# First attention steps of a fused attention, MLP and routed-experts kernel: who normalises the first step, in which order its heads and values are loaded, and where the third step's values stand

## The reference

```python
B, H, S, D = 4, 8, 576, 64                       # q, k, v
scores = q @ k.T / sqrt(D) - slope[h] * |i - j|  # only 0 <= i - j < 128, else -1e9
attn   = exp(scores - rowmax); attn /= attn.sum(-1) + 1e-9
x      = (attn @ v) as (2304 tokens, 512)
h      = x @ w_in                                # 512 -> 2048
x      = (h * clip(h + 3, 0, 6) / 6) @ w_out     # 2048 -> 512
e      = argmax(cosine(x, expert_emb) / tau)     # 8 experts, gate = softmax value of e
out    = gate * (relu(x @ w1[e]) @ w2[e])        # 512 -> 1024 -> 512
```

## Time and profile before

| | |
|---|---|
| median of 3 runs | 838.8 us (838.38 to 839.31) |
| the profiled execution | 838.55 us, of which the span from first to last instruction is 836.8 us |
| PE busy | 823.3 us, 98% of the span |
| DVE, ACT, POOL busy | 477.9, 395.8, 241.5 us |
| first matmul of the MLP | 22.18 us after the span's start |

### The profile page before, as it was taken

How to read it: one execution, slowest core, us unless ns; L and a number is a source line. 1 busy time by engine, 2 the same in 40 slices (tenths; PEclk the granted TensorE clock), 3 DMA queues, 4 the chain that set the end, 5 groups by cost and what they waited for, 6 DMA issues and landing times.

```text
span 836.8 us, 18599 instructions
## 1 busy us (share of the span) xinstructions
PE 823.3 (98%) x6533; PEld 707.0 (84%) x6533; DVE 477.9 (57%) x1469; ACT 395.8 (47%) x1057; POOL 241.5 (29%) x261
## 2 busy tenths in 40 slices
PE   7999999999999999999999999999999999999996
PEld 6888888888888888888888888888888888888885
DVE  7765575665766656756565578776543445554000
ACT  5674555545455455554554337533434334343442
POOL 5992000000000000000000101386665656666432
PEclk9999999999999999999999999999999999999999
DMA  8764211102112111121100026575555444552100
GB/s 243 226 190 152 77 52 58 33 15 76 52 41 69 33 40 51 52 76 35 32 13 2 27 88 168 167 224 176 165 161 169 128 140 140 164 157 66 50 14 11
DMA packets 54427, 80.18 MB, mean 96 GB/s; under 512 B 11752, under 2 KB 28136, under 8 KB 54210
## 3 DMA queue, kind: packets, MB, share of 16 engines
q1 hardware_dynamic: 47986, 67.57, 26.6%
q0 software_dynamic: 4000, 11.29, 4.2%
q10 hardware_dynamic: 2352, 0.14, 0.3%
HBM read 69.51 MB, written 11.30 MB: 97 GB/s over the span
## 4 chain that ended last, share of the span: by engine, by line
PE 94%; DMA 2%; DVE 2%; issue 0%; ACT 0%; SPq 0%; POOL 0%; POOLq 0%; ACTq 0%; DVEq 0%
PE ps_h L852 24%; PE ps_y L869 22%; PE ps_h L1004 16%; PE ps_s L1033 15%; PE ps_out L797 4%; PE ps_s L755 3%; PE ps_y L1028 3%; PE ps_out L1033 1%; PE ps_out L956 1%; DMA y_scratch<-gate_tok 1%; PE ps_s L774 1%; DMA arena<-in_k 1%; PE ps_s L780 1%; PE ps_s L777 1%; DMA en_all<-y_scratch,gather_ids 0%
## 5 line engine op out<-in xcount | busy, mean ns | idle before, releaser
L852 PE MATMUL ps_h<-x_hi,win_hi 128*128 128x256 f32 x576 | 165.6, 295 | 0.1
L852 PE MATMUL ps_h<-x_lo,win_hi 128*128 128x256 f32 x576 | 158.5, 283 | 0.0
L852 PE MATMUL ps_h<-x_hi,win_lo 128*128 128x256 f32 x576 | 158.3, 283 | 0.0
L1160 ACT CAST gated_hi<-gated 128x256 fp32r<-128x256 f32 x144 | 58.5, 406 | 138.3 <-PE ps_y L869 98.4
L1428 DVE TENSOR_TENSOR gated_lo<-gated,gated_hi 128x256 fp32r<-128x256 f32 x144 | 64.6, 449 | 101.9 <-ACT gated_hi L1160 101.9
L852 PEld LDWEIGHTS ps_h<-x_hi,win_hi 128*128 128x128 f32 x576 | 107.8, 190 | 8.3 <-issue 2.7
L869 PE MATMUL ps_y<-wout_hi,gated_hi 128*128 128x512 f32 x288 | 114.1, 396 | 0.0
L869 PE MATMUL ps_y<-wout_hi,gated_lo 128*128 128x512 f32 x288 | 113.8, 395 | 0.0
L628 POOL MEMSET arena<- 128x64 bf16 x2 | 0.2, 151 | 390.8 <-DVE x_lo L1402 390.8
L869 PE MATMUL ps_y<-wout_lo,gated_hi 128*128 128x512 f32 x288 | 112.1, 389 | 0.0
L852 PEld LDWEIGHTS ps_h<-x_hi,win_lo 128*128 128x128 f32 x576 | 107.9, 191 | 2.3
(11 more groups left out here) (241 smaller groups left out, 1563.7 us busy)
## 6 DMA issues: line engine op xcount, KB each, us to landing
arena<-in_moe_w SPq DMA_DIRECT2D x64, 512.0 KB, 4.2
arena<-in_v SPq DMA_DIRECT2D x40, 128.0 KB, 3.2
y_scratch<-y_sb SPq DMA_DIRECT2D x9, 512.0 KB, 3.8
en_all<-in_moe_w_in SPq DMA_DIRECT2D x16, 256.0 KB, 3.9
arena<-in_v SPq DMA_DIRECT2D x16, 256.0 KB, 3.2
en_all<-in_moe_w_out SPq DMA_DIRECT2D x16, 256.0 KB, 3.9
arena<-in_q SPq DMA_DIRECT2D x31, 128.0 KB, 2.4
arena<-in_k SPq DMA_DIRECT2D x31, 128.0 KB, 2.9
```

The costliest lines, as they stand in the source:

```text
L852: last = pe.matmul(ps_h[m % 2][:, 0:TB], a[:, c, w], r[:, c, x], start=n == 0, stop=n == 3 * KC - 1)
L1160: act.copy(gh[m % 2][:], gate[:]).then_inc(act_gh, 1)
```

## The change

ACT instead of DVE multiplies the probabilities of step 0 by the reciprocals (`normalise_first`). DVE still computes the reciprocals (`invert(0)`), now ahead of the last four biases. SP issues v of group 0 ahead of q and k of step 3, then two weight pieces, v of group 1, q and k of step 4, and two more weight pieces; `start_at_one` comes after all of these. On PE, the scores of step 4 go from iteration 2 to behind the transposes of step 2 in iteration 3, the values of step 2 go ahead of the transposes of step 3, and the idle transposes are 6 and 8 around the values of step 1 and 3 ahead of the values of step 3.

```diff
@@ load order, SP @@
             load_qk(1)
             load_qk(2)
-            start_at_one(sp, counting)
+            load_v(0)
             load_qk(3)
             for n in range(4):
+                if n == 2:
+                    load_v(1)
+                    load_qk(4)
                 sp.dma_start(w_raw[n], w_piece(n)).then_inc(ld_w[n], 16)
-                if n == 0:
-                    load_v(0)
-                    load_qk(4)
-            load_v(1)
+            start_at_one(sp, counting)
@@ transposes, PE @@
-                pe.wait_ge(dve_n, s + 1)
+                if s == 0:
+                    pe.wait_ge(act_n, 1)
+                else:
+                    pe.wait_ge(dve_n, s)
@@ main loop, PE @@
-                if 2 < it < FIRST:
-                    keep_busy((3, 14)[it - 3])
-                    if it == FIRST - 1:
-                        transposes(it - 1)
-                    values(it - OUT)
-                    if it == 3:
-                        keep_busy(8)
-                if 0 <= it - 1 < STEPS and it != FIRST - 1:
+                if it == 3:
+                    keep_busy(6)
+                    values(1)
+                    keep_busy(8)
+                if it == FIRST - 1:
+                    values(2)
+                if 0 <= it - 1 < STEPS:
                     transposes(it - 1)
                 if it == 2:
                     values(0)
+                if it == 3:
                     scores(4)
+                if it == FIRST - 1:
+                    keep_busy(3)
@@ ACT @@
+            def normalise_first():
+                act.wait_ge(dve_r, 1)
+                for n in range(4):
+                    a = columns_of(0, n)
+                    last = act.activation(a, a, ACT.Copy, scale=rinv[0:rows(0), 0, n:n + 1])
+                last.then_inc(act_n, 1)
...
+                if it == 1:
+                    normalise_first()
                 if 0 <= it - 1 < STEPS and it != FIRST - 1 and not turn_first:
                     take_pT(it - 1)
@@ DVE @@
-            def normalise(s):
+            def invert(s):
...
                 dve.reciprocal(rinv[0:R, b, :], rden[0:R, b, :]).then_inc(dve_r, 1)
+
+            def normalise(s):
+                R, b = rows(place(s)[0]), s % 2
+                invert(s)
                 dve.wait_ge(dve_r, s + 1)
...
                 if it == 1:
+                    invert(0)
                     bias_before(4, H)
-                    normalise(0)
```

More of the change, by code:

```diff
@@ L358, in _program @@
         pe_s, dve_s, act_e = sem("pe_s"), sem("dve_s"), sem("act_exp")
-        dve_d, dve_r, dve_n = sem("dve_den"), sem("dve_inv"), sem("dve_norm")
+        dve_d, dve_r, dve_n, act_n = sem("dve_den"), sem("dve_inv"), sem("dve_norm"), sem("act_norm_first")
         pe_t0, pe_t, act_t0, act_t, pe_o = sem("pe_t0"), sem("pe_t"), sem("act_t0"), sem("act_t"), sem("pe_o")
@@ L1364, in scores @@
                         op0=ALU.add, op1=ALU.min, accum_out=nmax[0:R, s % 2, n:n + 1]).then_inc(dve_s, 1)
-            def normalise(s):
-                g, i, q4 = place(s)
-                R, b = rows(g), s % 2
+            def invert(s):
+                R, b = rows(place(s)[0]), s % 2
                 dve.wait_ge(act_e, 4 * s + 4)
```

## The result

The changed kernel takes 843.2 us (median of 6 runs, 841.97 to 844.6) where the kernel before takes 838.8 (6 runs, 838.19 to 839.31). The ratio is 1.0054, 95% interval 1.0041 to 1.0067: 4.4 us slower. The forecast was 838.0 with a range to 839.6, so it was wrong, in sign and in size.

What follows compares the result with a forecast made beforehand. The prediction took PE's gapless matmul queue to bound the kernel, so its start sets the end. With the MLP at T + 10.54, 0.7 to 1.3 earlier, it took 0.8 off 838.55, giving 837.75, plus 0.25: 838.0, range 836.9 to 839.6.

Steps and rivals of the forecast that it cites:

- Bottleneck and method: Whole kernel: PE's gapless middle bounds it, so an earlier MLP start should move the end by as much.
- the sum: MLP start is T + 10.54: 21.5 at T = 10.95, 0.7 earlier, or 20.85 at T = 10.3, 1.3 earlier.
- T + 10.54: From DVE's scores of step 2 to the MLP's first matmul: 10.54 us, where it was 11.39 before.
- T: Start of DVE's scores of step 2: forecast 10.95 or 10.3, by the pace of PE's scores of step 3; before 10.79.
- the heads of step 3 come too late: Rival at PE's scores of step 3: k lands after 9.5, at 10.0 the MLP starts 0.5 later, 839.3; chance 0.14.
- The chance of the clock: At PE's start: standing still from about 7.5 to 8.8 may keep full clock away; counted by leaning to 0.8 gained.
- The rival on the clock: PE behind 15.7: half clock slows scores of step 4 and values of step 2; 0.45 slower, 839.2; chance 0.17.
- The three waits of 0.85: PE's order ahead of the MLP: waits of 0.49, 0.20 and 0.16 would go, with values of step 2 in front.
- ACT's normalising: Step 0 on ACT: four multiplications taking 1.15, ending at 9.6, freeing DVE at about 9.9 instead of 10.79.
- The gain in T (0.54): At DVE's scores of step 2: ACT's normalising brings them to 10.25, before the new load order takes part back.
- Weights, v, `start_at_one`: Loads ahead of the MLP: weight pieces in time with 3.3 of room, v early enough, moving `start_at_one` costs nothing.

Runs made afterwards that it cites:

- e4: The changed kernel with 3 and 6 idle transposes put into PE's gaps ahead of the scores of steps 2 and 3; 840.15 us, ratio 1.0023.
- e8: The changed kernel with the heads of step 3 loaded ahead of v of group 0 and idle transposes in PE's gaps; 839.15 us, ratio 1.0004.
- e1: The changed kernel with the load order of the kernel before; 841.69 us, ratio 1.0031.
- e6: The kernel before with only ACT's normalising of step 0 and the reciprocals ahead of the biases; 839.43 us, ratio 1.0015.
- e15: The changed kernel without all 17 idle transposes; 843.49 us, ratio 1.0057.
- e7: The changed kernel with the old load order and without the 6 and 8 idle transposes; 840.94 us, ratio 1.0018.
- e3: The changed kernel with the heads (q and k) of step 3 loaded ahead of v of group 0; 840.71 us, ratio 1.0012.
- e2: The kernel before with the new load order alone; 842.11 us, ratio 1.0040.
- e16: The changed kernel as it is, run again on another chip; 842.77 us, ratio 1.0041.
- e5: The kernel before with PE's new order alone, on the slower chip; 844.92 us, ratio 1.0009.
- e14: The kernel before with PE's new order alone, on a faster chip; 839.86 us, ratio 1.0004.

## Why the prediction was wrong

Bottleneck and method held: 4.71 of the 5.0 us lie ahead of the MLP's first matmul, and each row behind it moved along. The MLP starts 5.4 later than the 21.5 of the sum (26.89). Term by term:

- **T + 10.54, the failed step (3.7 of the 5.4).** It is T + 14.21. The prediction put it: "the 6 wait for DVE's scores of step 3 (T + 2.23) and are done before x_lo of step 0, the 8 run while DVE still normalises step 2 [...]: nothing of them is on the path." All its durations on PE behind T were those of full clock. At half clock DVE waited 0.88 for the transposes of step 1, and the transposes of step 2 started 1.47 after their turn (20.10, not 12.68 + 5.07 + 0.88 = 18.63), behind the values of step 1 and the 8. From there to the transposes of step 3 it took 3.70, not 2.54, and the rest 0.16 more. 0.88 + 1.47 + 1.16 + 0.16 = 3.67.
- **T, 1.7 of the 5.4.** T is 12.68, forecast 10.95. The scores of step 3 started at 9.90 and not at 8.8: k was issued at 6.15 instead of 5.9 and landed 3.6 later instead of 2.9. It lay inside my bounds (2.3 to 4.1), and I chose too near the lower one. k landed after the 9.5 at which the rival "the heads of step 3 come too late" sets in, so that rival's condition came true; but its price, 0.5 us, was worked out at full clock behind T and is a ninth of the loss. The other 0.63 is the transposes of step 0: from their start to T it took 1.29 at half clock, where I had 0.64 for them.
- **The chance of the clock.** The prediction named what happened, in one sentence: PE "now stands still from about 7.5 [...] to 8.8, and the full clock that the row shows behind 8.9 may not come". But it priced it as 0.7 on one block of scores and followed it no further. The rival on the clock looked only behind 15.7 and took full clock until then. (Its upper bound is also too low by its own terms: 2 times 1.08 is 0.66 above the 1.5 that gave 839.2, so 839.9 and not 839.7. The 843.2 lies beyond either.) e4 shows the size of what was left out: 2.9 us.
- **The three waits of 0.85.** Their working was right at full clock. In e8 x_hi of step 1 does not wait, and the transposes of step 3 start at 18.89, 0.15 after their turn (x_hi of step 1 at 15.97, + 0.80 + 1.74 + 0.23): the values of step 2 do fit in front. e8 starts the MLP at T + 11.35 and not T + 10.54 because of a new wait of 0.56 on DVE (next point), these 0.15, and 0.17 behind them (18.89 to 21.99 is 3.10 for 2.93); 0.07 were won in between.
- **ACT's normalising.** 1.26, forecast 1.15, as good as right. The gain in T (0.54) did not come: T is 10.78, 10.89 and 10.64 in e1, e6 and e8, against 10.79. PE's transposes of step 0 start behind ACT at 9.75 or so, and T is their end. And what the prediction did not follow is ACT's next piece: the copy of these transposes comes later too, and DVE's scores of step 3 wait for what stands behind it, so x_hi of step 0 is at T + 2.73 to 2.79.
- **Weights, v, `start_at_one`**: as forecast, without a wait ahead of the MLP.

The Trainium skill (TensorE: Matmul & The Clock Gate, Part 4: PE-mode transpose) says that transposes do not count for the full clock as other matmuls do. The runs do not agree. In the changed kernel PE ran from 16.02 to 21.52 almost only transposes, and the full clock came within the scores that followed; with the idle ones taken away, in e15, it came some 2 us later. In e1 it rose at 17.1, in the middle of 8 idle transposes, and in e7, without them, at 20.9. The values of step 1 stand among these transposes, so no run here has them alone.

The scatter fits the mechanism, though no run proves it: on e1's chip 32 of the 35 runs of the kernel before lie within 1.9 us (838.0 to 839.9, the other three at 841.5 to 843.6), while the 11 of e1 spread over 4.2 (839.6 to 843.8). What moves from run to run is presumably when the clock rises or falls among gaps that hang on DMAs.

## What to carry to other kernels

When PE waits at the start of a kernel, price a late load twice: once for the wait, and once with every PE duration behind it at half clock, until the trace shows what would bring the full clock back. A dependency queue worked out at full clock ("DVE is the queue, PE has slack") has to be worked out again at half clock before anything on PE is called off the path. Idle matmuls in a gap belong ahead of the work whose pace matters; on the path they cost their time, and taking them away may still gain nothing. And look which execution the trace is of: e1's was its fastest, e3's its slowest, so neither stands for its median.

## What the runs showed of the hardware

- The granted clock column reads 1.00 for the changed kernel up to 22 us while the same 24 matmuls take 1.56 instead of 0.84. The record seems to begin with its first change; until then the pace of matmuls of one shape is the clock to read.
- Once up, the clock fell to half again for a stretch in several kernels, behind pauses of PE: 12.1 to 15.6 before, 13.6 to 17.1 in e1, 15.1 to 18.5 in e4 (granted clock 0.50 between). Not every pause brings it: in e8 PE waited 1.35 ahead of the values of step 1 (14.37), and all behind ran at full pace.
- k of 128 KB behind 512 KB of v landed 3.6 after its issue (3.3 in e2, 3.5 in e16), against 2.3 behind heads alone.
- One chip of the four on which the experiments ran took 843.8 us for the kernel before, the others 838.9 to 839.1. Most of it lies behind the start: from the MLP's first matmul on, one kernel took 819.7 there (e5) and 814.9 on another chip (e14).
